# Routing in a fused attention and expert kernel: eleven chunks' gates ahead of the last chunk's, and expert 0's gather table apart

## The chip, the cores and the metric

The kernel runs on one core of a Trainium2 chip. The metric is the device time of one execution in microseconds (us). Three runs of the kernel before took 429.89, 430.24 and 430.44 us; the median is 430.24 us.

## The reference

Three stages follow each other. The first is a linear attention over 2 batches, 8 heads, 768 positions and 48 features, with a state that decays by `w`. Its output, as 1536 tokens of 384 values, goes into a layer of 8 experts; the third stage is a squared-ReLU network of 2048 hidden units. What matters here is how the experts' rows are chosen:

```python
logits = x @ w_gate                      # 1536 x 8
expert_idx = np.argmax(logits, axis=1)
for i in range(N):                       # in the order of the tokens
    e = expert_idx[i]
    if counts[e] < capacity:             # 384
        disp[e, counts[e]] = x[i]
        pos[i] = counts[e]
        counts[e] += 1
        keep[i] = True
h = np.maximum(np.einsum('ecd,edf->ecf', disp, w1), 0.0)
y = np.einsum('ecf,efd->ecd', h, w2)
out[i] = gate_w[i] * y[expert_idx[i], pos[i]]
```

The place of a token in its expert's list depends on all tokens before it, of both batches.

## The kernel before, in words

**The attention loop.** The tokens are worked in 12 chunks of 128 tokens (`NT` = 12, numbered 0 to 11), one chunk of batch 0 and one of batch 1 in turn. The order of work on each engine is written out by hand and held by semaphores. For each chunk TensorE makes scores, the state's part and the output (lines 497 to 544), ScalarE copies values and states and makes `cv` in eight pieces (`bonus`, line 768), VectorE masks the scores (`mask`, 952), makes keys and products (945, 937), adds the attention's rows into `x_sb` (`rows`, 962) and the heads' gate values into `heads_l` (`head_logits`, 965). GpSimd makes the decayed factors (415, 420), SyncE loads inputs and stores the rows to the scratch tensor `attention_out` (321). Behind each fourth chunk `logits` (970) sums the heads of four chunks into `L`.

**The routing.** After the last chunk VectorE takes the maximum of the logits (1004), subtracts it (1005) and makes the one-hot choice of an expert for all 12 chunks (1007 to 1009), then the last chunk's rows. TensorE turns the one-hots into positions (546 to 554): one product with the strictly triangular `before_b` counts within a chunk, twelve with `ones_b` over shifted slices of `oh` add the chunks before, and one adds each expert's region. These accumulate in one bank, `ps_pos`, which also holds the sums of the loop. VectorE splits a position into a row and a tile (1014 to 1021), makes `match` and `tokb` for all 8 experts (24 table columns, each twice: 1020, 1023) and twelve one-hot matrices (1026). TensorE multiplies these into the gather table (558), and VectorE makes the gather indices (1029, 1030), the largest count `peaki` (1033) and the experts' starts `starti` (1036).

**Into the experts.** GpSimd waits for the stored rows and for the indices, then gathers two tiles of expert 0 (429), zeroes a tile (436), and once it has read the largest count (290) gathers the rows of expert 1. Every engine branches on the largest count in `by_peak`; here it takes the side with 240 columns. TensorE then runs 18 filler products (`warm`, 617), transposes the gathered rows (666), runs 6 more fillers and starts expert 0's hidden layer (`hidden`, 577), whose products wait for the low part of the rows (`xs_ready`) column by column, and for the low part of the weights (`w_lo`). ScalarE copies the high part of the rows (847), VectorE makes the gate factors (`gates`, 1040 to 1044), the low part of the first weights (`split_lo`, 930) and then the low part of the rows (1131). Weights come in a ring of four units of 768 KB; SyncE loads unit 4 once both gathers have landed and the low part of unit 0 is made (359 to 362).

A step with `after(...)` counts a semaphore of its own engine and waits for it, so that the next instruction starts only when this one is done.

## Time and profile before

| | us |
|---|---|
| median of three runs | 430.24 |
| the profiled execution | 430.25 |
| its span | 428.4 |
| TensorE matmuls busy | 408.9 |
| VectorE busy | 257.2 |
| ScalarE busy | 217.7 |
| GpSimd busy | 66.0 |

The profile follows one execution. The span runs from its first to its last recorded instruction; 1.85 us of the execution lie around it. Matmuls overlap each other, and their ends are modelled. "Issue" is time in which an engine waited for nothing that the profile shows. The mean granted clock of TensorE is 0.976 of the full one. Times of the timeline count from the start of the span: the loop over the chunks ends at about 67 us, the experts run from 84 to about 225 us, and the squared-ReLU network from there to the end.

### The profile page before, as it was taken

Reading aid. Unit: us, or ns where it says so; the run is one execution under the profiler, and the core shown is the slowest. Engines: PE = TensorE matmul, PEld = TensorE weight load, DVE = VectorE, ACT = ScalarE, POOL = GpSimd, SP = SyncE. Lnnn points to the kernel's source line nnn. Section 1 sums busy time; section 2 is a strip of 40 time slices with the busy share of each in tenths; the row PEclk is TensorE's granted clock in tenths of the full one; section 3 lists DMA queues with packets and bytes.
Section 4 is the critical chain, followed back from the end, with each engine's and each line's share of the span. In section 5 each row is a group of like instructions: output and inputs, shape, how many; then the busy total and the mean of one; then the engine's idle time right before and its main releaser. Section 6 shows DMA issues by size and latency. Waiting matters only on the chain.

```text
span 428.4 us, 10138 instructions
## 1 busy us (share of the span) xinstructions
PE 408.9 (95%) x3966; PEld 378.4 (88%) x3966; DVE 257.2 (60%) x441; ACT 217.7 (51%) x430; POOL 66.0 (15%) x75
## 2 busy tenths in 40 slices
PE   7699995899999999999999999999999999999994
PEld 4699994699999999999988998899889989988984
DVE  6477767687886766777657553655455356536321
ACT  4577776146565564655536434454544445344320
POOL 3555450630201202000000000004000004000003
PEclk9899997699999999999999999999999999999998
DMA  7999982389746656546552332234223224100002
GB/s 211 245 264 286 245 304 101 109 296 387 244 179 237 218 166 230 213 154 220 176 195 73 94 129 75 73 129 165 73 79 141 75 73 145 77 2 0 0 2 80
DMA packets 18734, 66.02 MB, mean 154 GB/s; under 512 B 2888, under 2 KB 7641, under 8 KB 18704
## 3 DMA queue, kind: packets, MB, share of 16 engines
q1 hardware_dynamic: 16912, 60.93, 44.1%
q0 software_dynamic: 1792, 4.72, 2.9%
q8 instruction: 15, 0.25, 0.3%
q14 instruction: 15, 0.12, 0.1%
HBM read 59.35 MB, written 7.08 MB: 155 GB/s over the span
## 4 chain that ended last, share of the span: by engine, by line
PE 78%; DVE 4%; issue 1%; ACT 1%; POOL 0%; DVEq 0%; ACTq 0%; POOLq 0%
PE score_banks L577 19%; PE y_banks L577 18%; PE gate_bank L600 6%; PE spare_bank L600 6%; PE state_bank L600 6%; PE sum_bank L600 6%; PE gate_bank L590 5%; PE sum_bank L590 5%; PE state_bank L590 5%; PE spare_bank L617 1%; PE spare_bank L567 1%; DVE hlo L1100 0%; PE score_banks L558 0%; ACT cv L768 0%; DVE onehb L1077 0%
## 5 line engine op out<-in xcount | busy, mean ns | idle before, releaser
L930 DVE TENSOR_TENSOR wlo<-raw,whi 128x1536 fp32r<-128x1536 f32 x56 | 98.4, 1758 | 90.6 <-ACT whi L727 86.6
L727 ACT ACTIVATE whi<-raw 128x1536 fp32r<-128x1536 f32 x56 | 83.4, 1490 | 83.3 <-PE spare_bank L600 47.6
L458 POOL DMA_INDIRECT out<-osb,oidx x12 | 13.0, 1081 | 247.9 <-ACT osb L872 245.0
L1096 DVE TENSOR_TENSOR sq<-rl 128x512 f32<-128x512 f32 x48 | 32.9, 689 | 30.0 <-ACT rl L814 30.0
L429 POOL DMA_INDIRECT xg<-attention_out,gidx x16 | 19.5, 1220 | 83.1 <-PE spare_bank L567 64.1
L1100 DVE TENSOR_TENSOR hlo<-sq,hhi 128x512 fp32r<-128x512 f32 x48 | 30.9, 687 | 0.0
L577 PE MATMUL y_banks<-yhi,whi 128*128 (+1 forms) x72 | 28.4, 395 | 0.0
L577 PE MATMUL y_banks<-yhi,wlo 128*128 (+1 forms) x72 | 28.4, 395 | 0.0
L577 PE MATMUL score_banks<-ylo,whi 128*128 (+1 forms) x72 | 28.4, 395 | 0.0
L577 PE MATMUL score_banks<-yhi,whi 128*128 (+1 forms) x72 | 28.4, 395 | 0.0
L577 PE MATMUL score_banks<-yhi,wlo 128*128 (+1 forms) x72 | 28.4, 395 | 0.0
L577 PE MATMUL y_banks<-ylo,whi 128*128 (+1 forms) x72 | 28.4, 395 | 0.0
L814 ACT ACTIVATE rl<-y_banks 128x512 f32<-128x512 f32 x24 | 14.3, 599 | 27.6 <-PE y_banks L577 25.5
L814 ACT ACTIVATE rl<-score_banks 128x512 f32<-128x512 f32 x24 | 14.3, 601 | 26.9 <-PE score_banks L577 26.9
L817 ACT ACTIVATE hhi<-rl 128x512 fp32r<-128x512 f32 x48 | 27.5, 626 | 0.0
L577 PE MATMUL y_banks<-xshi,whi 128*128 128x240 f32 x96 | 26.4, 275 | 0.0
L577 PE MATMUL score_banks<-xshi,whi 128*128 128x240 f32 x96 | 26.4, 275 | 0.0
L577 PE MATMUL y_banks<-xshi,wlo 128*128 128x240 f32 x96 | 26.3, 274 | 0.0
L577 PE MATMUL score_banks<-xshi,wlo 128*128 128x240 f32 x96 | 26.3, 274 | 0.0
L577 PE MATMUL score_banks<-xslo,whi 128*128 128x240 f32 x96 | 26.3, 274 | 0.0
L577 PE MATMUL y_banks<-xslo,whi 128*128 128x240 f32 x96 | 26.3, 274 | 0.0
L768 ACT ACTIVATE cv<-vx,csum 128x56 f32<-128x56 f32 x96 | 23.6, 330 | 0.4
(221 smaller groups left out, 1137.8 us busy)
## 6 DMA issues: line engine op xcount, KB each, us to landing
raw<-in_wts SPq DMA_DIRECT2D x56, 768.0 KB, 4.4
tok<-in_tok SPq DMA_DIRECT2D x12, 384.0 KB, 5.6
feat<-in_feat SPq DMA_DIRECT2D x16, 192.0 KB, 4.5
vT<-in_vT SPq DMA_DIRECT2D x12, 192.0 KB, 4.2
attention_out<-x_sb SPq DMA_DIRECT2D x12, 192.0 KB, 4.7
out<-rl SPq DMA_DIRECT2D x12, 192.0 KB
feat<-in_feat SPq DMA_DIRECT2D x4, 448.0 KB, 8.2
xg<-attention_out,gidx POOLq DMA_INDIRECT x16, 4.4
```

The costliest lines, as they stand in the source:

```text
L429: nc.gpsimd.indirect_dma_start(out=xg[e % 2][:, q, :], out_offset=None, in_=xd[:, :], in_offset=bass.IndirectOffsetOnAxis(ap=gidx[:, e * C ...
L458: nc.gpsimd.indirect_dma_start(out=out[:, :], out_offset=bass.IndirectOffsetOnAxis(ap=oidx[:, t:t + 1], axis=0), in_=osb[:, t, :], in_offs ...
L577: mm = pe.matmul(banks[ft][:, 0:width], w[:, r, cols], x(k), start=(k == 0 and step == 0), stop=(k == KT - 1 and step == 2))
L590: mm = pe.matmul(ps_e[dt][:, 0:width], w[:, r, cols], x[:, par, ft, 0:width], start=(q == 0 and ft == 0 and step == 0), stop=(q == EQ - 1 ...
L600: mm = pe.matmul(ps_o[tt][:, 0:DM], x[:, par, ft, tt * P:(tt + 1) * P], w[:, r, cols], start=(v == 0 and ft == 0 and step == 0), stop=(v = ...
L727: return nc.scalar.activation(dst, src, ACT.Copy)
L768: ins = nc.scalar.activation(cv[n % 2][:, h, :], values(n % 2)[:, h, :], ACT.Copy, scale=csum[n % 2][:, h:h + 1])
L814: nc.scalar.activation(rl[:, ft, :], banks[ft][:, :], ACT.Relu).then_inc(h_relu, 1)
L817: nc.scalar.activation(hhi[:, par, ft, :], rl[:, ft, :], ACT.Square).then_inc(h_hi, 1)
L930: v.tensor_tensor(wlo[:, r, :], raw[:, r, :], whi[:, r, :].bitcast(F32), ALU.subtract).then_inc(w_lo, 1)
L1096: v.tensor_tensor(sq[:, ft, :], rl[:, ft, :], rl[:, ft, :], ALU.mult).then_inc(h_sq, 1)
L1100: v.tensor_tensor(hlo[:, par, ft, :], sq[:, ft, :], hhi[:, par, ft, :].bitcast(F32), ALU.subtract).then_inc(h_ready, 1)
```

## The change: what it does

The logits are summed in the loop: two chunks at a time behind every second chunk, chunk 10 and the last by themselves, and `L` now stands in the order of the batches. Behind chunk 10's rows (the eleventh of 12) VectorE takes maximum and difference of eleven chunks, and in the last chunk's turn it makes their one-hots (`oh_ready` 1). TensorE multiplies these into positions right behind the loop: twelve shifted products, `before_b` on eleven chunks and the region; only two products of 8 columns are left for the last chunk's one-hot (`oh_ready` 2). The gather table of expert 0 is made first, with 3 table columns instead of 24, in a bank of its own, and its indices are published as `gidx_ready` 1. The full table follows behind the largest count, and its indices for experts 1 to 7 come as `gidx_ready` 2, for which GpSimd waits before the gathers of expert 1. Filler products are redistributed: five between the two tables, five (for 18) ahead of the transposes and four (for 6) behind them, each with 512 columns instead of 288.

```diff
@@ gpsimd @@
+                    if e == 1:
+                        pool.wait_ge(gidx_ready, 2)
@@ tensor @@
+            def warm(count):
+                for _ in range(count):
+                    pe.matmul(ps_tr[:, :], ones_b[:, :], onehb[:, 0:4, :].rearrange("p t n -> p (t n)"), start=True, stop=True)
             pe.wait_ge(oh_ready, 1)
+            pe.wait_ge(csum_ready, NT + 1)
-            pe.matmul(ps_pos[:, 0:nt], before_b[:, :], oh[:, NT:2 * NT + 1, :].rearrange("p t e -> p (t e)"), start=True, stop=False)
-            for j in range(1, NT + 1):
-                pe.matmul(ps_pos[:, 0:nt], ones_b[:, :], oh[:, NT - j:2 * NT + 1 - j, :].rearrange("p t e -> p (t e)"),
-                               start=False, stop=False)
-            mm = pe.matmul(ps_pos[:, 0:NT * E], ones_b[:, :], region[:, :], start=False, stop=True)
+            final = NT - 1
+            for j in range(NT, 0, -1):
+                tiles = min(NT + 1, final + j)
+                pe.matmul(ps_pos[:, 0:tiles * E], ones_b[:, :], oh[:, NT - j:NT - j + tiles, :].rearrange("p t e -> p (t e)"),
+                               start=(j == NT), stop=False)
+            pe.matmul(ps_pos[:, 0:final * E], before_b[:, :], oh[:, NT:NT + final, :].rearrange("p t e -> p (t e)"), start=False, stop=False)
+            pe.matmul(ps_pos[:, 0:NT * E], ones_b[:, :], region[:, :], start=False, stop=False)
+            pe.wait_ge(oh_ready, 2)
+            pe.matmul(ps_pos[:, final * E:NT * E], before_b[:, :], oh[:, NT + final, :], start=False, stop=False)
+            mm = pe.matmul(ps_pos[:, NT * E:(NT + 1) * E], ones_b[:, :], oh[:, NT + final, :], start=False, stop=True)
             mm.then_inc(pos_psum, 1)
             for t in range(NT):
                 pe.wait_ge(onehot, t + 1)
+                mm = pe.matmul(ps_tab0[:, 0:2 * CT], onehb[:, t, :], tokb0[:, t, :, :].rearrange("p a s -> p (a s)"),
+                               start=(t == 0), stop=(t == NT - 1))
+            mm.then_inc(tab_psum, 1)
+            warm(5)
+            pe.wait_ge(tokb_ready, 1)
+            for t in range(NT):
                 mm = pe.matmul(ps_tab[:, 0:2 * E * CT], onehb[:, t, :], tokb[:, t, :, :].rearrange("p a s -> p (a s)"),
                                start=(t == 0), stop=(t == NT - 1))
             mm.then_inc(tab_psum, 1)
@@ first_rows @@
-                warm(18)
+                warm(5)
-                warm(6)
+                warm(4)
@@ scalar @@
-            act.wait_ge(shifted, 1)
+            act.wait_ge(shifted, 2)
@@ vector @@
+            def logits_of_pair(c):
+                dve.wait_ge(heads_ready, 2 * c + 4)
+                v.tensor_reduce(L[:, :, :].rearrange("p (b c) e -> p b c e", b=B)[:, :, c, :],
+                                heads_l[:, 2 * c:2 * c + 2, :, :].rearrange("p t h e -> p t e h"), AX.X, ALU.add).then_inc(logits_ready, 1)
+            def logits_of(n):
+                t = n % 2 * NC_ + n // 2
                 dve.wait_ge(heads_ready, n + 3)
-                v.tensor_reduce(L[:, n - 3:n + 1, :], heads_l[:, n - 3:n + 1, :, :].rearrange("p t h e -> p t e h"), AX.X, ALU.add).then_inc(logits_ready, 1)
+                v.tensor_reduce(L[:, t:t + 1, :], heads_l[:, n:n + 1, :, :].rearrange("p t h e -> p t e h"), AX.X, ALU.add).then_inc(logits_ready, 1)
+            def shift(lo, hi, count):
+                ts = slice(lo, hi)
+                after(v.tensor_reduce(r["mx"][:, ts], L[:, ts, :], AX.X, ALU.max))
+                v.tensor_tensor(Lm[:, ts, :], L[:, ts, :], be(r["mx"][:, ts], hi - lo), ALU.subtract).then_inc(shifted, 1)
+                dve.wait_ge(shifted, count)
+            def choose(lo, hi):
+                ts = slice(lo, hi)
+                after(v.scalar_tensor_tensor(cand[:, ts, :], Lm[:, ts, :], 0.0, bt(rev_e[:, :], E, hi - lo), ALU.is_equal, ALU.mult))
+                after(v.tensor_reduce(r["first"][:, ts], cand[:, ts, :], AX.X, ALU.max))
+                v.tensor_tensor(ohv[:, ts, :], bt(rev_e[:, :], E, hi - lo), be(r["first"][:, ts], hi - lo), ALU.is_equal).then_inc(oh_ready, 1)
             for n in range(NT):
                 mask(n)
                 keys(n)
                 if n + 1 < NT:
                     products(n + 1)
-                if n % 4 == 0 and n:
-                    logits(n - 1)
+                if n % 2 == 0 and n:
+                    logits_of_pair(n // 2 - 1)
+                if n == final:
+                    choose(0, final)
                 dve.wait_ge(y_done, n + 1)
                 dve.wait_ge(cv_ready, n + 1)
-                if n < NT - 1:
+                if n < final:
                     rows(n)
                 head_logits(n)
+                if n == final - 1:
+                    logits_of(n)
+                    dve.wait_ge(logits_ready, NC_)
+                    shift(0, final, 1)
+            logits_of(final)
+            dve.wait_ge(logits_ready, NC_ + 1)
+            shift(final, NT, 2)
+            choose(final, NT)
+            rows(final)
             dve.wait_ge(pos_psum, 1)
...
+            v.tensor_scalar(i12["tile"][:, :], bits, 7, P - 1, ALU.logical_shift_right, ALU.bitwise_and).then_inc(tiles_ready, 1)
+            dve.wait_ge(dve_step, steps.n)
             v.tensor_copy(r["pf"][:, :], i12["p"][:, :]).then_inc(dve_step, 1)
+            dve.wait_ge(tiles_ready, 1)
+            after(v.tensor_tensor(match0[:, :, :], bt(iota_s[:, 0:CT], CT), i12["tile"][:, :].unsqueeze(2).to_broadcast([P, NT, CT]), ALU.is_equal))
+            after(v.tensor_tensor(tokb0[:, :, :, :], match0[:, :, :].unsqueeze(2).to_broadcast([P, NT, 2, CT]),
+                                  token[:, :, 0:2].unsqueeze(3).to_broadcast([P, NT, 2, CT]), ALU.mult))
             for t in range(NT):
                 v.tensor_scalar(onehb[:, t, :], iota_p[:, :], r["pf"][:, t:t + 1], None, ALU.is_equal).then_inc(onehot, 1)
+            def gather_rows(table, cols):
+                w = cols.stop - cols.start
+                after(v.tensor_scalar(off[:, cols], table[:, 0:w], float(OUTSIDE), None, ALU.add))
+                v.tensor_tensor(gidx[:, cols], table[:, w:2 * w], off[:, cols], ALU.add).then_inc(gidx_ready, 1)
             dve.wait_ge(tab_psum, 1)
+            gather_rows(ps_tab0, slice(0, CT))
...
             v.tensor_copy(peaki[:, :], peak[:, :]).then_inc(count_ready, 1)
+            after(v.tensor_tensor(match[:, :, :], bt(iota_s[:, :], W_), i12["tile"][:, :].unsqueeze(2).to_broadcast([P, NT, W_]), ALU.is_equal))
+            v.tensor_tensor(tokb[:, :, :, :], match[:, :, :].unsqueeze(2).to_broadcast([P, NT, 2, W_]),
+                            token[:, :, 0:2].unsqueeze(3).to_broadcast([P, NT, 2, W_]), ALU.mult).then_inc(tokb_ready, 1)
...
             v.tensor_copy(starti[:, :], start[:, :]).then_inc(starti_ready, 1)
+            dve.wait_ge(tab_psum, 2)
+            after(v.tensor_scalar(off[:, CT:W_], ps_tab[:, CT:W_], float(OUTSIDE), None, ALU.add))
+            v.tensor_tensor(gidx[:, CT:W_], ps_tab[:, W_ + CT:2 * W_], off[:, CT:W_], ALU.add).then_inc(gidx_ready, 1)
```

## Rows read from the trace of the kernel before

**Rows 1.** The page, engines' busy time and share of the span.

```profile
PE 408.9 (95%) x3966; PEld 378.4 (88%) x3966; DVE 257.2 (60%) x441; ACT 217.7 (51%) x430; POOL 66.0 (15%) x75
```

**Rows 2.** Chain that ended last, 67 to 92 us: start us, us, what.

```profile
70.09 1.04 PE sum_bank L551 x12
...
76.71 1.04 issue
...
77.75 4.50 PE spare_bank L617 x18
...
84.26 2.11 PE score_banks L577 x18
```

**Rows 3.** Timeline of VectorE in the chunk loop: start us, us, what [idle before <-releaser].

```profile
28.07 1.29 DVE L952 TENSOR_TENSOR am<-score_banks,before 128x512 f32<-128x512 f32 x2
...
57.99 0.56 DVE L962 TENSOR_TENSOR x_sb<-y_banks,cv 128x384 f32<-128x384 f32 x1 [0.46 <-issue]
...
64.21 1.29 DVE L952 TENSOR_TENSOR am<-score_banks,before 128x512 f32<-128x512 f32 x2 [0.99 <-PE score_banks L505]
...
67.44 0.22 DVE L965 TENSOR_TENSOR heads_l<-y_banks,cv 128x64 f32<-128x64 f32 x1 [1.48 <-ACT cv L768]
```

**Rows 4.** Timeline of VectorE, last logits to the table's factors.

```profile
67.70 0.62 DVE L970 TENSOR_REDUCE L<-heads_l 128x32 f32<-128x256 f32 x1
...
69.51 0.26 DVE L1009 TENSOR_TENSOR oh<-rev_e,r_first 128x96 bf16<-128x96 f32 x1
...
69.69 0.55 DVE L962 TENSOR_TENSOR x_sb<-y_banks,cv 128x384 f32<-128x384 f32 x1
...
71.25 0.26 DVE L1014 TENSOR_TENSOR cand<-sum_bank,oh 128x96 f32<-128x96 f32 x1 [1.01 <-PE sum_bank L553]
...
72.11 0.46 DVE L1020 TENSOR_TENSOR match<-iota_s,i_tile 128x288 bf16<-128x288 f32 x1
...
72.69 0.75 DVE L1023 TENSOR_TENSOR tokb<-match,token 128x576 bf16<-128x576 bf16 x1
```

**Rows 5.** Timeline of VectorE, one-hots to the first expert's rows.

```profile
73.48 2.04 DVE L1026 TENSOR_SCALAR onehb<-iota_p,r_pf 128x128 bf16<-128x128 bf16 x12
...
76.06 0.18 DVE L1030 TENSOR_TENSOR gidx<-score_banks,off 128x24 uint32<-128x24 f32 x1
...
77.12 0.17 DVE L1036 CAST starti<-start 128x8 int32<-128x8 f32 x1
...
78.75 0.25 DVE L1040 TENSOR_REDUCE r_sum<-ex 128x12 f32<-128x96 f32 x1 [1.46 <-issue]
...
79.04 0.72 DVE L1042 TENSOR_SCALAR r_sum<-r_sum 128x12 f32<-128x12 f32 x1
...
80.31 1.76 DVE L930 TENSOR_TENSOR wlo<-raw,whi 128x1536 fp32r<-128x1536 f32 x1
...
83.55 0.42 DVE L1131 TENSOR_TENSOR xslo<-state_bank,xshi 128x256 fp32r<-128x256 f32 x1 [1.48 <-ACT xshi L727]
```

**Rows 6.** Timeline of GpSimd, the first gathers.

```profile
77.25 1.23 POOL L429 DMA_INDIRECT xg<-attention_out,gidx  x1 [16.12 <-DVE gidx L1030]
...
78.78 1.00 POOL L429 DMA_INDIRECT xg<-attention_out,gidx  x1 [0.31 <-issue]
...
80.38 2.56 POOL L429 DMA_INDIRECT xg<-attention_out,gidx  x1 [0.17 <-issue]
```

**Rows 7.** Timeline of ScalarE, the first copy of expert 0's columns.

```profile
83.13 0.38 ACT L727 ACTIVATE xshi<-state_bank 128x256 fp32r<-128x256 f32 x1 [11.17 <-PE state_bank L666]
```

**Rows 8.** The page, DMA issues: out<-in, queue, KB each, us to landing.

```profile
attention_out<-x_sb SPq DMA_DIRECT2D x12, 192.0 KB, 4.7
```

**Rows 9.** Windows of 1 us: us, busy (count) by engine, PEclk, DMA share, GB/s.

```profile
17.00:18.00 1.00, 0.18 (x4) 0.18 (x6) 0.92 (x2) 0.49 (x2) 0.00 (x0) 1.00 0.94 177
...
21.00:22.00 1.00, 1.00 (x26) 1.00 (x24) 0.34 (x2) 0.00 (x0) 0.60 (x1) 0.52 0.92 170
...
83.00:84.00 1.00, 1.00 (x9) 0.79 (x7) 0.45 (x2) 0.87 (x3) 0.75 (x1) 0.80 0.84 190
```

52 lines of the change are left out of this document (16 added, 36 removed).

## The prediction

> **What bounds the kernel now.** The page's busy shares come first: the matrix engine (PE) is busy 95% of the span [rows 1], so a change in the routing pays only where PE runs short of real work. The chain that ended last shows the place: between the last chunk and the first expert it leaves PE for VectorE (DVE), comes back for fourteen small multiplications into the positions, goes to DVE again, and then holds PE for 1.04 us of "issue" and 4.50 us of 18 filler multiplications, before the first expert's products at 84.26 us [rows 2]. The filler is not work: the timelines say what is late. DVE walks from the last logits (67.70) to the last gather indices (76.06) with two waits for PE [rows 4, 5]; GpSimd (POOL) starts the first gather at 77.25 [rows 6]; the first copy of gathered columns is at 83.13 on ScalarE (ACT) [rows 7], and the first low part at 83.55 on DVE, which had been idle 1.48 us for it [rows 5]. From 84.26 PE runs nearly without a gap, so what the hand-over saves comes off the end, and this is the quantity to work out: how much earlier than 83.55 can xslo start. The sum is made against the profiled execution's 430.25 us (span 428.4), which is the median of the runs (430.24) to a hundredth.
>
> **The chunk loop.** Two reductions of 256 elements per lane (0.62 us) become five of 128; bounds are 0.25 (96 elements) and 0.62 [rows 4, 5], I take 0.33. In most chunks DVE idles 0.46 us before x_sb, and the 0.33 hides there [rows 3]. In the third chunk DVE is late: the mask at 28.07 starts with no idle ahead of it [rows 3], so up to 0.33 is exposed; PE's own work covers part. I take 0.1 lost, with ends 0 and 0.33. Without the cover, five exposed reductions would cost 1.65, less about 1.2 for the two taken out. Behind chunk 10's row stand the logits, maximum and shift of eleven chunks: 0.20 + 0.25 + 0.26 and three steps of 0.03 between dependent operations = 0.8 us, in DVE's idle 0.99 us before the mask at 64.21 [rows 3]. If it overran by 0.3, that mask would be late, but chunk 11 waits for ACT: DVE idles 1.48 us before 67.44 for cv [rows 3]. In that idle time the choice for eleven chunks (three operations, 0.29 apart, 0.87 us) fits. Cost nothing.
>
> **Last logits to positions.** Now: from 67.70 to the one-hot at 69.51, 1.81 us [rows 4]. After: the last chunk alone, one reduction of 64 elements (0.20) and four operations of 8 elements (0.17, the conversion at 77.12 [rows 5]), each with 0.03 to the next: 0.23 + 4 x 0.20 = 1.03, so the one-hot starts at 68.73. PE meanwhile, free since its last chunk, has added the 12 shifted products (1.04 us now [rows 2]), the first `before_b` product and the region ahead of time; of the fourteen, behind the one-hot stand two of 8 columns. Then x_sb is late next: 0.55 us, starting 0.1 after the one-hot (now 69.69 [rows 4]), ends at 69.38, and PE's two products are done beside it. So cand goes from 71.25 [rows 4] to 69.40: 1.85 us saved. The x_sb step also starts the last store on SP's queue, 0.85 earlier; POOL waits for its landing.
>
> **Positions to first indices.** From cand to match 0.86 us, unchanged but 0.02 for the conversion put ahead (70.28). match0 has 36 elements for 288, tokb0 72 for 576: bounds 0.17 and 0.25, I take 0.20 each against 0.46 and 0.75 [rows 4, 5]; with the steps the one-hots start at 70.75, not 73.48 [rows 5]: 2.73 saved. Their 2.04 us stay, and PE follows each with 6 columns instead of 48, 0.05 less at the end. First indices at 73.28, not 76.06, first gather at 74.47, not 77.25 [rows 5, 6]: **2.78 us saved there**.
>
> **What is added behind it.** On DVE's queue, ahead of the branch: match (0.50 with its step) and tokb (0.75) of the full table, then a wait for PE's second table and two more operations. From 73.28: the count's three operations to 73.84, match to 74.34, tokb to 75.09, starts to 75.78. PE has put 5 fillers of 512 columns (2560 columns, 2.13 us at 1.2 GHz, from 73.1) ahead of its wait, so it begins the second table at 75.2. Twelve products of 48 columns: at most 0.087 each (1.04 over 12 with 104 columns [rows 2]), at least half that; I take 0.06, 0.7 us, done 75.95. Second indices end at 76.4, against 77.29 for the start conversion, which is last now [rows 5]. So the branch, gates and first split are only 0.9 earlier: 1.46 to the gates (77.85), 1.56 for them, 1.76 for the split (78.75 to 80.31 to 82.07 now [rows 5]), ending at 81.17. Queued behind DVE's new wait are those gates and the split, and for the split wait PE's first hidden product and SP's next weight load (0.9 earlier; the ring holds four units). POOL's new wait for the second indices is met at 76.4, before its zeroing of 0.44 us behind the second gather ends at about 77.7; ACT's wait for the starts is met at 75.8, and its copies come at 80.
>
> **Who is last at xslo.** By PE: branch 1.04 after the table (76.95), 5 fillers (79.1), six transposes, and ACT's first copy 80.2 to 80.6. By gathers: the second now lands before its transposes, so 2.5 earlier it is there by 80.1, and the copy is done by 81.0 at latest. By DVE: split until 81.17. DVE is last, by 0.2 to 0.6 us; its idle 1.48 is used up. xslo 81.17 against 83.55: **2.38 us saved**, not 2.78.
>
> **The POOL port.** Two rows show DVE and POOL holding each other. The 12-element r_sum at 79.04 takes 0.72, not 0.17, and ends at 79.76, as POOL's gather of 78.78 + 1.00 does; the gather of 80.38 takes 2.56 and ends at 82.94, 0.87 behind the split of 80.31 + 1.76 [rows 5, 6]. After: the first gather (74.47) meets tokb until 75.09 and ends at 75.96, 0.26 late, which is hidden (80.1 above has it). r_sum starts at 78.14, inside expert 1's first gather, from about 77.85 for 1.0: held 0.6, as now 0.55. I leave gates at 1.56; ends 1.0 (nothing held) and 2.5 (held by a gather as long as 2.56). The Trainium skill (SBUF — State Buffer, "Who interferes with whom") lets a tensor_scalar in a two-port mode and a GpSimd operation block each other wholly, which agrees with 79.04; but it infers that a two-input tensor_tensor does not stall a gather's descriptors, and the gather at 80.38 under the split speaks against that. By its inference the first gather would end 0.26 earlier, and the sum would be the same.
>
> **The clock.** Fillers began at 77.75 and the granted clock was half until 83.4 (0.80 in 83 to 84) [rows 2, 9]: up after 5.65 us of unbroken work. At the start, work resumed at 17.8 and it was up at 21.96 [rows 9]: 4.15. Counted from 76.95, the rise is at 81.1 to 82.6; if the short pause before does no harm, from 73.1, at 77.3 to 78.8. First hidden product: xslo 0.42 + 0.15 = 81.75. Cold work behind that costs half its time, 0 to 0.45; I take 0.1. The Trainium skill (TensorE: Matmul & The Clock Gate, "What's actually happening") has the throttled clock as the default state, released by sustained activity; that speaks against this change, which spends fewer filler columns (2560 + 2560 + 2048 for 5184 + 1728, but split by a pause), and is the last rival below.
>
> **Sum.** 2.38 - 0.1 (loop) - 0.1 (clock) = 2.2 us: 430.25 - 2.2 = **428.05 us**, 0.5% faster.
>
> **Rivals.** (A) *PE or gather last, DVE freed.* If nothing holds r_sum and the second table is quick, DVE gains up to 0.9 more, and ACT's copy decides, done at 80.6 by PE's chain above: xslo at 80.64, 2.9 us earlier, 427.3. For: 0.72 is mostly a held operation; against: expert 1's gather moves with it. Chance 0.15. (B) *The hand-over is held on DVE or in the loop.* r_sum held for 2.5 instead of 1.56, or the reductions exposed, or cold work of 0.45: gain 0.9 to 1.5, 429.1. A variant is the last store: at its usual 4.7 us to landing [rows 8] from 69.4 it ends at 74.1, later than the indices at 73.46, and delays the gather by 0.65, still covered. Chance 0.17. (C) *It doesn't do what it says:* the early part is right, but something behind it (branch, gates) starts no earlier, since the second table comes at 77.3 instead of 76.4: gain 0.3 to 0.8, about 429.7. Against: PE has only 0.7 us of products behind 75.2. Chance 0.05. (D) *Slower by the clock.* The pause behind the second table undoes the first fillers and the five after it are too few to bring the clock up: PE then runs the first products at half rate. Each us cold behind 81.75 costs 0.5; the 2.4 saved is used up when the rise comes after 86.6, and the other side begins there. A rise at 89 costs 3.6, giving 431.5. For: the pause; against: 86.6 is 9.6 us behind 76.95, where 5.65 was enough. Chance 0.03.
>
> **The numbers.** The forecast's chance is 0.60. What a measurement can tell from no change is about 0.2%, 0.86 us: slower takes (D), 0.03; the same takes (C) and a scrap of (B), 0.07; faster the rest, 0.90. Range: (A) below to 427.2, (B) above with both its causes together to 429.3; outside are (C), (D) and half of the tails.
>
> **What would show it.** Right: cand near 69.4, first gather near 74.5, xslo near 81.2 with no idle before it, PE's first xshi product near 81.8, and from there the same spacing as now. Wrong: DVE idle at cand for PE; r_sum over 1.5 us; fillers ending after xslo; PEclk at 0.5 behind 82.6; x_sb of the third chunk later with every later chunk late too.

## The result, and the profile after

Twenty executions of the changed kernel have a median of 427.84 us (425.29 to 430.48), twenty of the kernel before 429.9 (428.39 to 431.62). The ratio is 0.9959, 95% interval 0.9942 to 0.9976: 1.8 us faster, 1.0 to 2.5. A second set of twelve gave 0.9966 (0.9945 to 0.9987). The three executions known ahead of the prediction had hidden how wide both kernels spread.

The profiled execution of the change took 430.48 us, with a span of 428.7: it is the longest of its twenty, and no shorter than the profile of before. That is what makes this case instructive, since its trace shows the gain and also the place where it was given back. The granted clock of TensorE (PE) on its page, in forty slices:

```profile
PEclk9899998599999999999999999999999999999999
```

The clock line is lowest in its eighth slice of 10.7 us (75 to 86 us), at a half: that is where the first expert begins. Next the timeline of VectorE (DVE) through the hand-over, for [rows 3 to 5]:

```profile
68.05 0.23 DVE L982 TENSOR_TENSOR heads_l<-y_banks,cv 128x64 f32<-128x64 f32 x1 [0.69 <-ACT cv L785]
...
69.96 0.25 DVE L1043 TENSOR_TENSOR cand<-sum_bank,oh 128x96 f32<-128x96 f32 x1
...
71.32 2.04 DVE L1057 TENSOR_SCALAR onehb<-iota_p,r_pf 128x128 bf16<-128x128 bf16 x12
...
73.84 0.16 DVE L1062 TENSOR_TENSOR gidx<-score_banks,off 128x3 uint32<-128x3 f32 x1
...
74.86 0.76 DVE L1070 TENSOR_TENSOR tokb<-match,token 128x576 bf16<-128x576 bf16 x1
...
76.59 0.18 DVE L1077 TENSOR_TENSOR gidx<-score_banks,off 128x21 uint32<-128x21 f32 x1
...
77.66 0.25 DVE L1081 TENSOR_REDUCE r_sum<-ex 128x12 f32<-128x96 f32 x1 [0.90 <-issue]
...
77.95 0.54 DVE L1082 TENSOR_SCALAR r_sum<-r_sum 128x12 f32<-128x12 f32 x1
...
78.99 1.76 DVE L947 TENSOR_TENSOR wlo<-raw,whi 128x1536 fp32r<-128x1536 f32 x1
...
81.86 0.42 DVE L1171 TENSOR_TENSOR xslo<-state_bank,xshi 128x256 fp32r<-128x256 f32 x1 [1.11 <-ACT xshi L744]
```

The loop ended 0.61 us later than in the profile of before (last head logits at 68.05, not at 67.44), so differences are taken from that instruction. The cand row comes 1.91 behind it, where it came 3.81 behind [rows 3, 4]: 1.90 saved, and DVE no longer waits for PE there. Not all of it is the change's. In the profile of before the clock fell at 69.7, just ahead of the first product of the positions (69.83):

```profile
69.00:70.00 1.00, 0.17 (x3) 0.18 (x4) 0.93 (x4) 1.00 (x2) 0.00 (x0) 0.87 0.00 0
```

Where the same routing met the full clock (the experiments with fillers alone below), cand came 3.24 behind, so 1.33 of the 1.90 are the shorter path and 0.57 the clock. The first indices come 5.79 behind, not 8.62 [rows 3, 5]: 2.83 saved. xslo comes 13.81 behind, not 16.11 [rows 3, 5]: 2.30 saved, yet DVE is idle 1.11 us ahead of it. Then the timeline of GpSimd (POOL), which answers to [rows 6]:

```profile
75.01 1.70 POOL L433 DMA_INDIRECT xg<-attention_out,gidx  x1 [13.70 <-DVE gidx L1062]
...
77.02 1.00 POOL L433 DMA_INDIRECT xg<-attention_out,gidx  x1 [0.31 <-DVE gidx L1077]
```

And the timeline of PE in the same stretch:

```profile
69.64 0.18 PE L568 MATMUL sum_bank<-oh,before_b 128*128 128x8 bf16 x1 [0.95 <-DVE oh L1016]
...
76.73 2.31 PE L555 MATMUL spare_bank<-onehb,ones_b 128*128 128x512 bf16 x5 [0.39 <-issue]
...
79.37 0.48 PE L683 MATMUL state_bank<-ident,xg 128*128 128x128 f32 x1 [0.34 <-DMA xg<-attention_out,gidx]
...
80.92 0.48 PE L683 MATMUL state_bank<-ident,xg 128*128 128x128 f32 x1 [0.65 <-DMA xg<-attention_out,gidx]
...
81.62 1.91 PE L555 MATMUL spare_bank<-onehb,ones_b 128*128 128x512 bf16 x4
...
86.68 0.27 PE L599 MATMUL y_banks<-xshi,whi 128*128 128x240 f32 x1
...
88.69 0.60 PE L589 MATMUL spare_bank<-ident,xg 128*128 128x128 f32 x4
```

The first gather takes 1.70 us instead of 1.23; it was issued while DVE's multiplication `tokb` ran (74.86 to 75.62). The second starts at 77.02, and PE idles 0.34 us for the first and 0.65 for the second. In the chain that ended last, for [rows 2], the second gather stands as an item of its own, behind it four fillers of 0.43 us each, and behind them the first hidden product, most of it at half rate (3.31 us instead of 2.11):

```profile
77.02 3.86 DMA xg<-attention_out,gidx
...
81.83 1.71 PE spare_bank L555 x4
...
83.53 3.31 PE score_banks L599 x18
```

The windows of 1 us show the clock that goes with it (columns as in [rows 9]):

```profile
72.00:73.00 1.00, 1.00 (x7) 0.62 (x7) 1.00 (x8) 0.24 (x1) 0.00 (x0) 0.74 0.00 0
...
86.00:87.00 1.00, 1.00 (x10) 1.00 (x10) 0.59 (x2) 0.12 (x1) 0.00 (x0) 0.93 0.66 203
```

It fell at 72.5 and rose at 86.1, where in the profile of before it had risen at 83.4 [rows 9], ahead of the first product. The places to compare with in PE's timeline of before are the second hidden product and the first transposes of expert 1:

```profile
86.40 0.38 PE L577 MATMUL y_banks<-xshi,whi 128*128 128x240 f32 x1
...
88.52 0.60 PE L567 MATMUL spare_bank<-ident,xg 128*128 128x128 f32 x4
```

The second hidden product starts 18.63 us behind the last head logits, in the kernel before 18.96; the transposes 20.64, before 21.08. Of the 2.30 us saved at xslo, 0.33 and then 0.44 are left. The rest was lost to fillers and products at 1.2 GHz. With the loop's end 0.61 later and 0.13 more behind the hand-over, that makes the span 0.3 us longer than before.

### The profile page after: what moved, and what is told of

Same layout as the page of the kernel before. It is cut to its first block, busy times and chain, and to the rows that moved or that the text cites. A ratio compares the mean times of both kernels' runs of the same rounds, so it can differ in the third digit from the quotient of the medians.

```text
span 428.7 us, 10159 instructions
## 1 busy us (share of the span) xinstructions
PE 413.1 (96%) x3970; PEld 378.8 (88%) x3970; DVE 259.8 (61%) x454; ACT 217.5 (51%) x430; POOL 65.8 (15%) x75
## 4 chain that ended last, share of the span: by engine, by line
PE 76%; DVE 4%; issue 2%; ACT 1%; DMA 1%; DVEq 0%; POOL 0%; ACTq 0%; POOLq 0%
PE score_banks L599 19%; PE y_banks L599 17%; PE gate_bank L622 6%; PE spare_bank L622 6%; PE state_bank L622 6%; PE sum_bank L622 6%; PE gate_bank L612 5%; PE sum_bank L612 5%; PE state_bank L612 5%; PE spare_bank L589 1%; DMA xg<-attention_out,gidx 1%; PE spare_bank L555 1%; DVE ylo L1159 0%; DVE hlo L1140 0%; PE score_banks L574 0%
## 5 line engine op out<-in xcount | busy, mean ns | idle before, releaser
L599 PE MATMUL score_banks<-xshi,whi 128*128 128x240 f32 x96 | 27.4, 285 | 0.0
```

The lines of the kernel that those rows point to most:

```text
L599: mm = pe.matmul(banks[ft][:, 0:width], w[:, r, cols], x(k), start=(k == 0 and step == 0), stop=(k == KT - 1 and step == 2))
```

## The experiments

Each kernel was timed beside the kernel before. The column of the hand-over is the time from the last head logits to the first transposes of expert 1 in the one profiled execution, the last column how many executions have a mean granted clock under 0.980 and the range of that mean. From these transposes to the end of the span every profiled execution takes 339.6 to 340.0 us, so whatever separates them lies in the chunk loop or in the hand-over.

| kernel | median us (executions) | ratio to before, 95% interval | hand-over us | mean clock |
|---|---|---|---|---|
| before | 429.87 as a mean (103) | | 21.08 | 0.971 to 0.987, 60 of 103 under 0.980 |
| the change, first set | 427.84 (20) | 0.9959 (0.9942 to 0.9976) | 20.64 | 0.978 to 0.991, 6 |
| the change, second set | 428.60 (12) | 0.9966 (0.9945 to 0.9987) | 18.05 | 0.978 to 0.991, 4 |
| fillers bridged | 427.89 (10) | 0.9951 (0.9929 to 0.9974) | 18.40 | 0.980 to 0.990, 0 |
| table apart only | 429.22 (12) | 0.9978 (0.9957 to 0.9999) | 20.38 | 0.977 to 0.990, 3 |
| choice ahead only | 428.06 (12) | 0.9947 (0.9926 to 0.9969) | 18.69 | 0.979 to 0.986, 3 |
| before, change's fillers | 429.98 (12) | 0.9997 (0.9977 to 1.0016) | 21.38 | 0.971 to 0.982, 10 |
| reductions by four | 428.01 (12) | 0.9952 (0.9928 to 0.9975) | 18.20 | 0.978 to 0.991, 3 |
| factors in three | 427.60 (12) | 0.9961 (0.9934 to 0.9987) | 18.10 | 0.978 to 0.990, 3 |
| bridged and three | 427.79 (12) | 0.9954 (0.9930 to 0.9978) | 17.61 | 0.980 to 0.991, 0 |
| all three | 426.98 (7) | 0.9930 (0.9900 to 0.9960) | 18.32 | 0.983 to 0.990, 0 |
| **clock kept up** | **426.81 (6)** | **0.9913 (0.9888 to 0.9939)** | 17.68 | 0.988 to 0.995, 0 |
| pairs in the old loop | 429.61 (12) | 0.9982 (0.9964 to 1.0000) | 20.84 | 0.975 to 0.987, 7 |
| before, clock kept up | 428.82 (12) | 0.9979 (0.9955 to 1.0003) | 20.19 | 0.985 to 0.996, 0 |

Theory 1: the change shortens the path as forecast, and what an execution keeps of it depends on when the granted clock rises. Theory 2: the landing of the second gather alone decides.

**The change again.**

> The change itself again, beside the others of this call. Both theories: about 1.8 us faster than the kernel before (ratio 0.993 to 0.998). Theory 1 (the clock): most of the spread between its executions is the time at which the granted clock rises, because TensorE's fillers are broken by the wait for the second gather of expert 0; so executions with a mean clock near 0.978 are 2 to 3 us longer than those near 0.990. Theory 2 (the gather): the landing of that gather alone sets the time, and the clock's mean and the time have nothing to do with each other.

Its profile has the same rows up to the gathers, but the clock was up in time. First the timeline of PE:

```profile
76.78 1.68 PE L555 MATMUL spare_bank<-onehb,ones_b 128*128 128x512 bf16 x5 [0.40 <-issue]
...
78.91 0.33 PE L683 MATMUL state_bank<-ident,xg 128*128 128x128 f32 x1 [0.45 <-DMA xg<-attention_out,gidx]
...
80.46 0.33 PE L683 MATMUL state_bank<-ident,xg 128*128 128x128 f32 x1 [1.00 <-DMA xg<-attention_out,gidx]
...
84.04 0.38 PE L599 MATMUL y_banks<-xshi,whi 128*128 128x240 f32 x1
...
86.16 0.60 PE L589 MATMUL spare_bank<-ident,xg 128*128 128x128 f32 x4
```

And its windows of 1 us:

```profile
77.00:78.00 1.00, 1.00 (x4) 0.39 (x3) 0.25 (x2) 0.00 (x0) 0.94 (x1) 0.65 0.47 92
...
78.00:79.00 1.00, 0.55 (x4) 0.09 (x2) 0.90 (x4) 0.00 (x0) 0.84 (x3) 1.00 0.57 160
```

PE waited even longer for the second gather (1.00 us, since its work was done sooner), and still the second hidden product began 15.93 us behind the last head logits (at 68.11), not 18.63. Of these 2.70 us, 0.52 are the gathers: issued at the same place, both landed that much sooner (first transposes 10.80 behind, not 11.32, the second tile's 12.35, not 12.87), and no run shows why. The other 2.2 are the clock, 0.16 of it ahead of xslo. PE's pauses for the gathers were of the same kind in both profiles, and the clock rose at 77.7 in one and at 86.1 in the other, so the pauses alone do not decide it.

The mean granted clock of a whole execution is a blunt measure of this: it is 0.979 in the first of these profiles and 0.980 in the second. In the second the clock was also low for 6.8 us in the chunk loop (3.4 in the first) and for 2.6 us at the very end, where nothing was seen to wait for it. Over all 32 executions of the change, the 10 with a mean clock under 0.980 have a mean of 429.6 us and the 12 at 0.985 and above one of 426.9. This is a correlation, and it doesn't say in which stretch the clock was low. Theory 1 expected it; theory 2's half, that clock and time have nothing to do with each other, falls, though the landing of the gathers has its own part.

**Fillers without a pause.**

```diff
-                warm(5)
+                warm(6)
                 for q in range(2):
+                    if q == 1:
+                        warm(2)
...
-                warm(4)
+                warm(2)
```

> The change with its fillers set so that TensorE has no pause: six ahead of the transposes of the first tile, two between those of the first and second tile, two behind. One filler more in all. Theory 1 (the clock): unbroken work from about 76.7 us, so the rise comes 1.5 to 4 us sooner than in the change, and the first hidden product starts at about 82.4 on its operands, not at 83.5 behind fillers: 1 to 2.5 us faster than the change (ratio to the kernel before 0.990 to 0.994), and mean clocks of 0.978 are gone. Theory 2 (the gather): the landing is where it was; within 0.4 us of the change (ratio near 0.996).

In this kernel's profile the fillers do not do what they were set for. The clock had risen at 75.1, ahead of them, so they ran fast and PE still idled for both gathers:

```profile
77.70 0.33 PE L685 MATMUL state_bank<-ident,xg 128*128 128x128 f32 x1 [1.03 <-DMA xg<-attention_out,gidx]
...
79.23 0.33 PE L685 MATMUL state_bank<-ident,xg 128*128 128x128 f32 x1 [0.55 <-DMA xg<-attention_out,gidx]
```

The clock stayed up all the same. Mean clocks under 0.980 are gone (0 of 10, and 0 of 12 in the later kernel with the same fillers, where the change has 10 of 32), as theory 1 said, but only just: nine of these 22 stand at 0.980. The gain in time stayed below its forecast: the two bridged sets have a mean of 427.8 us over 22 executions, the change 428.2 over 32, and the intervals of the ratios overlap. That the lowest mean clocks go away was shown; a gain of 1 us or more was not.

**One part at a time.** The table apart without the early choice:

```diff
-                if n == final:
-                    choose(0, final)
...
-            logits_of(final)
-            dve.wait_ge(logits_ready, NC_ + 1)
-            shift(final, NT, 2)
-            choose(final, NT)
+            logits_of_pair(NC_ - 1)
+            dve.wait_ge(logits_ready, NC_)
+            shift(0, NT, 1)
+            choose(0, NT)
```

> One part alone: expert 0's table apart and the change's fillers, but maximum, difference, choice and positions for all twelve chunks behind the loop, as before (the logits are still summed in pairs of chunks in the loop). By the steps of the prediction: first gather 0.9 us earlier than before, and for the full table's extra operations the split of the first weights ends about 1 us later than in the kernel before; so xslo gains at most 0.4. Theory 1: with the clock late in a third of the executions the median is 0 to 1 us slower than the kernel before (ratio 1.000 to 1.003). Theory 2: 0.4 us faster (0.999).

The ratio, 0.9978, is 0.9 us below the kernel before; theory 1 had expected no gain and lies just outside the interval, theory 2's 0.4 us inside. xslo came 14.54 us behind the last head logits, 1.57 sooner than before, where 0.4 at most had been expected. Little of that is the table: in the kernel before with only the new fillers (below) it came at 14.62. There the first gather started 9.22 behind and here 8.07, yet its rows were in use at 13.04 there and at 13.11 here; 0.47 of the 1.15 us went into the longer gather, and what took the rest isn't shown. The trace also shows the clock working against the fillers, first in the timeline of PE:

```profile
78.33 1.25 PE L555 MATMUL spare_bank<-onehb,ones_b 128*128 128x512 bf16 x5 [0.55 <-issue]
...
81.49 0.34 PE L682 MATMUL state_bank<-ident,xg 128*128 128x128 f32 x1 [1.91 <-DMA xg<-attention_out,gidx]
```

And in its windows of 1 us:

```profile
78.00:79.00 1.00, 0.67 (x4) 0.32 (x5) 0.18 (x2) 0.00 (x0) 0.69 (x2) 0.87 0.31 53
...
81.00:82.00 1.00, 0.51 (x3) 0.51 (x4) 1.00 (x1) 0.00 (x0) 0.70 (x2) 0.84 0.27 46
```

Here the clock rose at 78.3, beside the five fillers; they were done in 1.25 us instead of 2.1, PE idled 1.91 us for the gather, and the clock fell again at 81.7, just ahead of the products that needed it, until 85.1. The choice ahead without the table:

```diff
-            gather_rows(ps_tab0, slice(0, CT))
+            gather_rows(ps_tab, slice(0, W_))
...
-                warm(5)
+                warm(18)
```

> The other part alone: logits in the loop, choice and positions of eleven chunks ahead, but one full table and the fillers of the kernel before (18 and 6 of 288 columns). By the prediction's step the gathers come 1.85 us earlier, and everything behind them moves with it: theory 1: 1.5 to 1.9 us faster than the kernel before (ratio 0.9955 to 0.9965), so nearly all that the whole change gives. Theory 2: the same 1.85, and the whole change is better by 0.3 to 0.6. If the reductions in the loop cost their full 0.3 each in chunks 2 and 4, 1.2 us faster (0.997).

0.9947: at least as good as the whole change, so the table apart adds nothing that these runs can show. The trace tells why. The gathers in the timeline of POOL in this kernel:

```profile
75.73 1.23 POOL L433 DMA_INDIRECT xg<-attention_out,gidx  x1 [14.12 <-DVE gidx L1052]
...
77.26 1.00 POOL L433 DMA_INDIRECT xg<-attention_out,gidx  x1 [0.31 <-issue]
```

With one full table the first gather starts 7.89 us behind the last head logits and the second 9.42; in the change 6.96 and 8.97. The first is 0.93 earlier by the small table, the second only 0.45, since the first one takes 1.70 for 1.23 beside the full table's multiplication. The second is the one that PE waits for in the change. In this kernel PE waits for neither: the 18 fillers end at 80.51, 12.67 behind, where the change's second gather landed at 12.87 and 12.35. xslo came 13.76 behind here, 13.81 and 13.13 in the two profiles of the change.

**The fillers alone,** in the kernel before:

```diff
-                    pe.matmul(ps_tr[:, 0:E * CT * NT], ones_b[:, :], match[:, :, :].rearrange("p t s -> p (t s)"), start=True, stop=True)
+                    pe.matmul(ps_tr[:, :], ones_b[:, :], onehb[:, 0:4, :].rearrange("p t n -> p (t n)"), start=True, stop=True)
...
-                warm(18)
+                warm(5)
...
-                warm(6)
+                warm(4)
```

> The kernel before with nothing but the change's fillers ahead of and behind the transposes (five and four of 512 columns for eighteen and six of 288). Theory 1 (the clock): the five end about 2.4 us before the eighteen did, TensorE then pauses about 1.2 us for the first gather and again for the second, so the clock rises 2 to 5 us later than in the kernel before and the four cold fillers delay the first product by 0.9: 1 to 2.5 us slower than before (ratio 1.0025 to 1.006), mean clocks of 0.972 in many executions. Theory 2 (the gather alone): the second transposes come when they came; within 0.3 us (ratio 0.9993 to 1.0007).

The ratio is 0.9997: theory 1's 1 to 2.5 us slower did not come. Theory 2's ratio did, but not by its reason, since the second tile's transposes come 1.49 sooner. The trace shows two effects that cancel. The first transposes in the timeline of PE:

```profile
80.18 0.48 PE L666 MATMUL state_bank<-ident,xg 128*128 128x128 f32 x1 [1.02 <-DMA xg<-attention_out,gidx]
```

And xslo in that of DVE:

```profile
81.76 0.42 DVE L1131 TENSOR_TENSOR xslo<-state_bank,xshi 128x256 fp32r<-128x256 f32 x1 [0.59 <-ACT xshi L727]
```

PE waits for the first gather, and xslo is 14.62 us behind the last head logits instead of 16.11. Of these 1.49 us, 0.59 are faster positions, since the clock fell later in this execution (first indices at 8.03, not 8.62); 0.90 were the eighteen fillers, which in the kernel before had ended later than the gather landed. Against that the first hidden product took 3.63 us to the second instead of 2.28, at 1.2 GHz, and its start slipped to 1.12 behind xslo, not 0.57: 10 of 12 executions have a clock under 0.980.

**The reductions in the loop.** Four chunks at a time for the first eight, in the change:

```diff
-                if n % 2 == 0 and n:
-                    logits_of_pair(n // 2 - 1)
+                if n in (4, 8):
+                    logits_of_four(n // 2 - 2)
+                if n == 10:
+                    logits_of_pair(4)
```

> The change with the logits of chunks 0 to 7 summed four chunks at a time in chunks 4 and 8, as in the kernel before, one pair in chunk 10. Theory A (the reductions cost in the early chunks, where VectorE has no idle time): no reduction in chunk 2, and the masks from chunk 2 to chunk 5 take 13.5 us; 0.1 to 0.5 us faster than the change. Theory B (the loop's end moves by 0.8 us either way with the loads, and the reductions are hidden): no difference that can be measured.

And pairs in the kernel before:

```diff
-                if n % 4 == 0 and n:
+                if n % 2 == 0 and n:
                     logits(n - 1)
```

> The kernel before with its logits summed by pairs in the loop (chunks 2, 4, 6, 8, 10) and the last pair behind it. The last reduction has 128 elements instead of 256 and saves 0.24 us of the hand-over. Theory A (a reduction in chunk 2 delays the loop): masks from chunk 2 to chunk 5 take up to 14.9 us instead of 13.5, and the time is 0 to 0.4 us longer than before (ratio 1.000 to 1.001). Theory B (hidden): 0.2 to 0.3 us shorter (0.9993 to 0.9997).

Masks 2 to 5 took 14.90 us in the first profile of the change, but 13.52 in its second and 13.52 with reductions by four; in the old loop with pairs 13.55, and without them, in the kernel with only new fillers, 14.17. The long ones stand where GpSimd's multiplications meet DVE's (a product of 0.69 takes 1.67), and that moves with the loads from one execution to the next, with the reductions or without. In time the reductions by four can't be told from the change (0.9952). The time with pairs is 0.8 us shorter, not longer (0.9982, interval 0.9964 to 1.0000), theory B's 0.2 to 0.3 among it. Theory A's longer masks did not come, and its time lies at the edge of the interval or outside.

The last head logits stand between 65.99 and 68.38 us over all profiled executions, and a part of that spread is the clock again, while the second chunk (number 1) is worked. The extremes are the kernel before with the clock kept up (below) and the change with reductions by four. Their windows of 1 us, in this order:

```profile
18.00:19.00 1.00, 1.00 (x46) 1.00 (x43) 0.02 (x1) 1.00 (x6) 0.95 (x1) 1.00 0.95 281
...
18.00:19.00 1.00, 1.00 (x23) 1.00 (x21) 0.00 (x0) 0.00 (x0) 0.48 (x1) 0.50 1.12 382
```

And the mask of chunk 2 in their timelines of DVE, which in the second waits 2.79 us for PE:

```profile
20.74 1.29 DVE L963 TENSOR_TENSOR am<-score_banks,before 128x512 f32<-128x512 f32 x2 [0.47 <-PE score_banks L505]
...
23.53 1.29 DVE L969 TENSOR_TENSOR am<-score_banks,before 128x512 f32<-128x512 f32 x2 [2.79 <-PE score_banks L511]
```

From the mask of chunk 1 to that of chunk 2 pass 5.06 us in the one profile in which the clock did not fall there, 6.56 to 7.63 in the six in which it was low for 3.4 us, and 7.77 to 8.61 in the seven in which it was low for 6.8. The last head logits stand at 65.99, at 67.2 on the mean and at 67.9. No kernel here was made to change it.

**The gather's hold.**

```diff
-            v.tensor_tensor(tokb[:, :, :, :], match[:, :, :].unsqueeze(2).to_broadcast([P, NT, 2, W_]),
-                            token[:, :, 0:2].unsqueeze(3).to_broadcast([P, NT, 2, W_]), ALU.mult).then_inc(tokb_ready, 1)
+            for s in range(0, NT, 4):
+                v.tensor_tensor(tokb[:, s:s + 4, :, :], match[:, s:s + 4, :].unsqueeze(2).to_broadcast([P, 4, 2, W_]),
+                                token[:, s:s + 4, 0:2].unsqueeze(3).to_broadcast([P, 4, 2, W_]), ALU.mult).then_inc(tokb_ready, 1)
```

> The change with the full table's tokb made by three multiplications of four chunks instead of one of twelve. Port theory: the first gather reads its indices while a two-input multiplication holds the port; with pieces of 0.27 us it gets in between, so it takes 1.2 to 1.45 us instead of 1.70 and the second gather starts 0.25 to 0.45 earlier; the median gains 0.2 to 0.4 us on the change. Rival (the 1.70 is the price of a first gather beside any work): 1.70 stays.

The timeline of POOL in this kernel:

```profile
74.68 1.31 POOL L433 DMA_INDIRECT xg<-attention_out,gidx  x1 [12.90 <-DVE gidx L1062]
...
76.29 1.00 POOL L433 DMA_INDIRECT xg<-attention_out,gidx  x1 [0.31 <-issue]
```

1.31 us instead of 1.70, and the second gather starts 8.54 behind the last head logits, not 8.97, so 0.43 us earlier: both as the port theory had it. All profiles agree: 1.70 or 1.71 in the five with the multiplication whole beside the first gather, 1.30 or 1.31 in the four with three pieces, 1.22 or 1.23 in the five with none beside it. They show that the length of the multiplication sets the hold; that a port is the reason is inferred. In time it can't be told from the change (0.9961).

With the bridged fillers besides (both edits above):

> Fillers without a pause (as in e1_bridged) and tokb in three pieces together. If both theories hold: 0.3 us faster than e1_bridged, 427.3 to 427.8 us against 429.9 before (ratio 0.993 to 0.995), no execution with a mean clock below 0.980. If the gather's hold is not what the bridged version waits for: the same as e1_bridged.

17.61 us is the shortest hand-over of all profiles, and no clock is under 0.980; the median, 427.79, is that of the bridged kernel. The hold is worth too little to be seen in the time.

**Together, and the clock kept up.** The three edits (bridged fillers, factors in three, reductions by four) in one kernel:

> The change with bridged fillers, tokb in three pieces and the early logits summed by four: the parts that looked good, together. Clock theory and port theory: 17.6 us or less from the last head logits to the first transposes of expert 1 (18.05 to 20.64 in the change), no mean clock below 0.980, median 427.0 to 427.8 us (ratio 0.992 to 0.995). Rival (the loop's end and the rise decide by chance, the parts do nothing): as the change, 0.996 to 0.997.

The ratio is 0.9930 and the median 426.98, as forecast, with no clock under 0.983; the hand-over of the profiled execution, 18.32 us, is not the 17.6 that was expected. Its timeline of PE says why:

```profile
75.76 2.74 PE L555 MATMUL spare_bank<-onehb,ones_b 128*128 128x512 bf16 x6 [0.39 <-issue]
...
78.29 0.42 PE L685 MATMUL state_bank<-ident,xg 128*128 128x128 f32 x1
...
79.65 0.27 PE L685 MATMUL state_bank<-ident,xg 128*128 128x128 f32 x1
```

The clock was low until 79.5, so six fillers took 2.74 us, and the two sets of transposes waited for fillers and for no gather: 11.31 and 12.67 behind the last head logits, where the profile of bridged and three, with the clock up at 77.3, has 10.44 and 11.84. A count that is right at one level of the clock is too long or too short at the other. Then fillers in every gap of PE (`early` is `warm` with `ones_b` for both operands):

```diff
+            early(3)
             pe.wait_ge(oh_ready, 2)
...
             mm.then_inc(pos_psum, 1)
+            early(7)
             for t in range(NT):
+                if t:
+                    early(1, 1)
...
-            warm(5)
+            warm(8)
...
-                warm(6)
+                warm(7)
...
-                        warm(2)
+                        warm(6)
...
-                warm(2)
+                warm(3)
```

> The same, and TensorE given fillers in every gap from the end of the loop: three ahead of the last one-hot, seven behind the positions, one of 128 columns with each one-hot, eight between the tables, seven, six and three around the transposes. Clock theory: the granted clock does not fall behind the loop, so nothing of the hand-over or the first products is cold: mean clock 0.988 to 0.996, the spread between executions halves, and the median is 0.5 to 1.5 us below c1_all_three: 426 to 427 us (ratio 0.990 to 0.993). If the clock falls all the same, the longer fillers delay the second table by up to 2 us and the time is 0.5 to 2 us above c1_all_three. Rival (the clock is not what separates the executions): within 0.3 us of c1_all_three with the same spread.

The timeline of PE in this kernel:

```profile
78.56 0.33 PE L694 MATMUL state_bank<-ident,xg 128*128 128x128 f32 x1
...
81.54 0.35 PE L608 MATMUL score_banks<-xshi,whi 128*128 128x240 f32 x1 [0.16 <-DVE xslo L1191]
...
85.90 0.60 PE L598 MATMUL spare_bank<-ident,xg 128*128 128x128 f32 x4
```

And the windows of 1 us:

```profile
77.00:78.00 1.00, 0.98 (x5) 0.51 (x6) 0.24 (x1) 0.00 (x0) 1.00 (x2) 1.00 0.67 181
...
82.00:83.00 1.00, 1.00 (x11) 1.00 (x11) 1.00 (x2) 0.18 (x1) 0.69 (x2) 1.00 0.91 362
```

The granted clock is full from 23 us to the end of the span, PE waits for neither gather, and the first products run at full rate. The hand-over, 17.68 us, is all the same no shorter than the 17.61 of bridged and three, whose clock was low for 6.8 us in the routing: there the low clock cost nothing that the hand-over shows. The ratio is 0.9913 (0.9888 to 0.9939), 3.7 us below the kernel before, its interval just clear of the change's. The standard deviation of its six executions is 1.1 us, against 1.4 of the change and 1.5 of all three: smaller, not half. The 0.5 to 1.5 us against the kernel with all three are not settled by six and seven executions: the medians are 0.2 us apart, which is what the rival said, the means 0.4 (426.7 and 427.1). This is the version that beats both kernels, by several edits at once.

**The clock without the change,** in the kernel before:

```diff
+            early(10)
             pe.wait_ge(oh_ready, 1)
...
             mm.then_inc(pos_psum, 1)
+            early(12)
             for t in range(NT):
+                if t:
+                    early(1, 1)
...
-                warm(18)
+                warm(11)
                 for q in range(2):
+                    if q == 1:
+                        warm(2)
...
-                warm(6)
+                warm(4)
```

> The kernel before with nothing but fillers: ten behind the loop, twelve behind the positions, one of 128 columns with each one-hot, eleven, two and four of 512 columns around the transposes, in place of eighteen and six of 288. The routing is as before. Clock theory: the granted clock does not fall, the positions take 0.5 us less, the transposes no longer wait for fillers, nothing of the first products is cold: 19.4 to 20.0 us from the last head logits to the first transposes of expert 1 where the kernel before has 21.08, so 1.1 to 1.7 us faster than before (ratio 0.996 to 0.9975), as much as the whole change gives. Rival (the change's gain is its shorter path and the clock is a bystander): within 0.4 us of the kernel before.

0.9979, 0.9 us faster, with an interval that reaches from none to 1.9. All clocks are 0.985 and above, though in the profiled execution the clock still fell at 76.3, behind PE's 1.94 us of issue ahead of the branch, and the hand-over was 20.19 us, a little above what was expected. The clock alone thus gives about half of what the change gives, not as much, and the interval does not exclude none. With the clock kept up on both sides the shorter path stands out best: 17.68 us of hand-over against 20.19, medians of 426.81 and 428.82, though the faster of the two also has its factors in three and its reductions by four.

## Why the prediction was right, and where it was wrong

The forecast was 428.05 us, the median is 427.84; the move against the measured kernel before is 1.8 us where 2.2 were worked out, and the median lies inside the stated range. That it came within 0.2 us is luck: the second set has 428.60, and single executions spread over 5 us. Point by point:

- **The chunk loop** (0.1 lost): the overrun before the mask did not come, DVE kept 0.18 us of idle time there, and the choice hid in the wait for `cv`. The reductions cost nothing that the runs show. The loop's end moves by 2.4 us between profiles for other reasons, in part the clock in its second chunk, and that was not in the sum.
- **Last logits to positions** (1.85): 1.90. x_sb was late next, as said. 0.57 of the saving came from a profile of before whose positions stood at the low clock; against one at the full clock it is 1.33.
- **Positions to first indices** (2.78): 2.83, with the same 0.57 in it.
- **Second indices at 76.4,** or 8.96 behind the last head logits: 76.77, 8.72 behind. But from there to the gates were 0.90 us, not 1.46. The step took the idle time ahead of the gates in [rows 5] as the price of the branch whatever came before; 0.56 of it were not paid. That the largest count had been known for 2 us by then is the likely reason, and wasn't tried by itself. The gates took 1.33 us for 1.56. So the split ended 12.7 us behind, where 13.73 were forecast: 0.24, 0.56 and 0.23 too long.
- **Who is last at xslo:** the step that failed. DVE was named, with the gather hidden and no idle time ahead of xslo; it was the second gather, with DVE idle 1.11 and 0.77 us, in both profiles of the change. DVE's part was priced 1.03 too high in the first profile and 1.37 in the second. The gather's part, "the copy is done by 81.0 at latest", is 13.56 behind the last head logits, and xslo came at 13.81 and 13.13, so that bound was about right, but its two halves were not: the 0.26 us of hold, called hidden, were 0.47 and in the path, and the landing was bounded by transposes that had waited for fillers, which left room of about 0.9 us that a slower landing then used up. The 2.38 us saved at xslo came out as 2.30 in one profile and 2.98 in the other, so the number survived a wrong mechanism.
- **The POOL port:** r_sum took 0.54 and 0.17 in the two profiles, at the seam between a gather and the zeroing of a tile, not inside a gather of expert 1; why it was held once and not the other time isn't shown. The gather under `tokb` was held 0.47, for 0.26 forecast, and the three pieces show that the hold follows the multiplication. The third gather, which took 2.56 where the split started 0.07 us ahead of it, took 1.01 in both: the split no longer starts ahead.
- **The clock** (0.1): the term that was mis-sized. "Counted from 76.95, the rise is at 81.1 to 82.6" supposed that the rise follows the start of the work by 4.15 to 5.65 us. In the two profiles of the change it came 9.4 and 0.9 us behind the start of the last five fillers, so that count doesn't hold. It is worth nothing in one profile and 2.0 in the other (from xslo to the second hidden product 2.80 and 4.82 us, 2.85 in the kernel before). On the mean it is at most about 1.3 us, if the 12 executions with the best clocks (426.9) are set against all 32 (428.2), and that holds what the clock costs in the loop too. Two signs of being wrong that the prediction named came in the first profile: the clock at a half behind 82.6, and fillers that end behind xslo. Rivals (B) and (D) named the mechanism; it took part of the gain and left the median on the side that was forecast.

The mean price of the clock and the clock's share of the loop's spread stay estimates from groups of executions; only profiled executions show the clock's place.

## What to carry to other kernels

When a path ahead of dense products gets shorter, look at what the matrix engine does in the shorter time: fillers sized for the old path either hold the work up (0.9 us in the kernel before) or end early and leave PE idle (1.91 us with the table apart only, behind which the clock fell again). Which it is depends on the clock that they meet, and a late rise cost 2.0 us in one profile of the change and nothing in the other. Compare more than one profiled execution from the last common instruction, and read in which stretch the clock was low, before a difference of half a per cent is explained; the mean clock does not tell the stretch. Splitting a result so that its first part comes early pays only if the last transfer that the consumer needs comes early too.

## What the runs showed of the hardware

- A gather whose issue falls on a DVE multiplication with two inputs in SBUF is held: 1.70 us behind one of 0.76, 1.31 behind three of a third each, 1.23 with none. The Trainium skill ("SBUF — State Buffer", "Who interferes with whom") infers that such an operation doesn't hold a gather's descriptors; here the gather is held, whichever part of it is.
- The granted clock fell again behind a pause of 1.91 us that followed quickly run fillers (at 81.7 in the kernel with the table apart only), and did not behind pauses of 1.03 and 1.00 us. Five fillers that take 2.31 us at 1.2 GHz took 1.25 when the clock rose beside them, so a count that bridges a wait at 1.2 GHz leaves a pause at 2.4.
- The same program takes 425.3 to 430.5 us in twenty executions. The clock's part stands in two places: in the second chunk of the loop (5.1 to 8.6 us from one mask to the next) and behind the routing (15.93 and 18.63 us to the second hidden product).
- Two gathers issued at the same place landed 0.52 us apart in two executions of one program, with no reason that a row shows.
